# Attention, dense layer and routed experts on one core: the dense result made transposed, and routed rows kept as 16-bit planes that the DMA turns

## What is computed

```python
# attention in chunks of 64 positions: q, k, v are (4, 8, 576, 64)
scores = scale * np.matmul(q_c, k_c.transpose(0, 1, 2, 4, 3))
attn = softmax(scores)
x = np.matmul(attn, v_c)                 # as (2304, 512)
# dense layer, d_ff = 2048
h = x @ w_in
x = (h * np.clip(h + 3.0, 0.0, 6.0) / 6.0) @ w_out
# eight experts, two for each token, d_ff = 1024
noisy_logits = x @ w_gate + np.log1p(np.exp(x @ w_noise)) * noise
for e in range(8):
    for k in range(2):
        mask = top2[:, k] == e
        h = np.maximum(x[mask] @ w1[e], 0.0)
        out[mask] += top2_w[mask, k, None] * (h @ w2[e])
```

## Time and profile before

| | |
|---|---|
| median of three executions | 1008.01 us |
| the profiled execution's own time | 1007.72 us |
| its span, first to last instruction | 1005.9 us |
| TensorE clock granted, mean | 0.999 of full speed |
| TensorE busy | 978.1 us, 97% of the span |
| GpSimd busy | 481.8 us, 48% |
| VectorE busy | 466.1 us, 46% |
| ScalarE busy | 331.6 us, 33% |
| DMA | 141.31 MB, 140 GB/s mean |

### The profile page before, as it was taken

How to read it: one execution, slowest core, us unless ns; L and a number is a source line. 1 busy time by engine, 2 the same in 40 slices (tenths; PEclk the granted TensorE clock), 3 DMA queues, 4 the chain that set the end, 5 groups by cost and what they waited for, 6 DMA issues and landing times.

```text
span 1005.9 us, 18539 instructions
## 1 busy us (share of the span) xinstructions
PE 978.1 (97%) x5823; PEld 825.3 (82%) x5824; DVE 466.1 (46%) x878; ACT 331.6 (33%) x468; POOL 481.8 (48%) x743
## 2 busy tenths in 40 slices
PE   6999999999999999999999999999999999999996
PEld 6888888888988988988877878878787887888885
DVE  5554455455456456463555533433344343433344
ACT  3322333332342342332423333333333333333332
POOL 5995000100100200597562876848487584933345
PEclk9999999999999999999999999999999999999999
DMA  9352132232332322624375565656556565337629
GB/s 343 127 180 74 43 106 76 103 106 75 106 105 75 105 75 95 231 84 167 122 221 140 133 186 151 177 128 185 167 128 174 155 184 132 94 94 177 168 78 350
DMA packets 135675, 141.31 MB, mean 140 GB/s; under 512 B 96192, under 2 KB 96320, under 8 KB 135616
## 3 DMA queue, kind: packets, MB, share of 16 engines
q1 hardware_dynamic: 111376, 74.73, 25.9%
q0 software_dynamic: 12288, 44.05, 13.9%
q10 hardware_dynamic: 11952, 21.76, 7.0%
HBM read 77.07 MB, written 40.63 MB: 117 GB/s over the span
## 4 chain that ended last, share of the span: by engine, by line
PE 56%; POOL 35%; issue 4%; DMA 3%; POOLq 1%; DVE 1%; ACT 0%; SPq 0%; ACTq 0%; DVEq 0%
PE ps L1265 15%; POOL W L507 11%; PE ps L1252 11%; PE ps L1384 10%; PE ps L1279 10%; POOL W L503 8%; PE ps L1283 5%; POOL W L456 5%; POOL W L453 3%; POOL W L524 2%; POOL y_hi L544 2%; POOL W L521 1%; PE ps L1301 1%; POOL EXraw L490 1%; POOL routed_x L466 1%
## 5 line engine op out<-in xcount | busy, mean ns | idle before, releaser
L1384 PE MATMUL ps<-W,hT_part 128*128 (+1 forms) x1032 | 251.1, 398 | 2.4 <-ACT hT_part L749 1.2
L1252 PE MATMUL ps<-W,xg_part 128*128 (+1 forms) x1032 | 249.2, 396 | 4.3 <-POOLq L514 3.5
L1252 PEld LDWEIGHTS ps<-W,xg_part 128*128 128x128 f32 x1032 | 192.6, 187 | 52.9 <-issue 6.7
L1384 PEld LDWEIGHTS ps<-W,hT_part 128*128 128x128 f32 x1032 | 191.2, 189 | 45.0 <-issue 3.1
L1265 PE MATMUL ps<-x_part,W 128*128 128x384 f32 x1152 | 222.8, 342 | 3.8 <-POOL W L456 3.1
L1265 PEld LDWEIGHTS ps<-x_part,W 128*128 128x128 f32 x1152 | 200.1, 188 | 11.1 <-POOL W L456 5.4
L466 POOL DMA_INDIRECT routed_x<-x,slot_blk x36 | 36.1, 1002 | 310.8 <-DVE slot_blk L908 216.8
L507 POOL TENSOR_TENSOR W<-EXraw,W 128x256 fp32r<-128x256 f32 x224 | 164.0, 763 | 4.7
L1279 PE MATMUL ps<-W,g_part 128*128 128x512 f32 x576 | 149.9, 395 | 0.0
L503 POOL TENSOR_SCALAR W<-EXraw 128x256 fp32r<-128x256 f32 x224 | 106.5, 502 | 83.0 <-PE ps L1384 75.3
L1279 PEld LDWEIGHTS ps<-W,g_part 128*128 128x128 f32 x576 | 106.7, 188 | 17.8
(11 more groups left out here) (185 smaller groups left out, 792.3 us busy)
## 6 DMA issues: line engine op xcount, KB each, us to landing
EXraw<-in_w POOLq DMA_DIRECT2D x24, 1024.0 KB, 5.9
QKV<-qkv SPq DMA_DIRECT2D x15, 768.0 KB, 4.5
routed_y<-y_sb ACTq DMA_DIRECT2D x43, 256.0 KB, 4.7
routed_y<-zero_tile SPq DMA_DIRECT2D x14, 768.0 KB, 3.8
xg<-routed_x ACTq DMA_DIRECT2D x40, 256.0 KB, 2.9
Wraw<-w_moe SPq DMA_DIRECT2D x16, 512.0 KB, 8.2
EXraw<-in_w SPq DMA_DIRECT2D x8, 1024.0 KB, 6.3
out<-y_lo SPq DMA_DIRECT2D x18, 256.0 KB, 4.5
```

Source lines behind the costliest of these rows:

```text
L1252: last = nc.tensor.matmul(dst, a(ha), b(hb), start=(i == 0), stop=(i == n - 1))
L1384: last = nc.tensor.matmul(ps[:, 4, :], hT_part[hh][:, n, :], W[hw][:, weights(slot, W1W + n * DM, DM)], start=(n == 0 and k == 0), stop=(n ...
```

## The change

The dense layer's `down` makes x1 transposed (features x tokens): the weights become the stationary operand and g the moving one, 12 matmuls of 384 columns instead of 9 of 512, into four banks (2 to 5). Attention and gate move to banks 6 and 7. The accumulators are copied to one `x1T` (ACT two pieces of 384, DVE one of 768), and the logits read it directly; `x1_transpose` and its copies are gone. For the scatter DVE writes each tile of x1T as 16-bit planes (`halve_x1`), SP turns it by a DMA transpose (`turn_rows`), and POOL scatters the turned planes, so that `routed_x` holds planes. SP reads each expert tile from DRAM with one DMA transpose (`turn_early`, `turn_x`, two or three tiles ahead), DVE puts the planes together in `xT` (`merge_x`), and `xg_high` and `xg_low` read `xT` in SBUF; `xg_transpose`, `load_rows` and `x_residual` are gone. Tiles 0 to 2 wait for the scatters of blocks 0 to 3 alone, but the first `xg_high` waits for block 4's scatter, whose source it overwrites. g32 has one buffer. The blocks are written out in place of the loop. The gate of block 4, which runs in the last block, moves two slices forward.

```diff
-            run(0, 0, 0, 0, False, True)
-            with engine.Fori(0, (NB - 2) // 2) as w:
-                run(2 * w + 1, 1, 3 * w, 3, True, True)
-                run(2 * w + 2, 0, 3 * w, 6, True, True)
-            run(NB - 1, 1, 3 * ((NB - 2) // 2), 3, True, False)
+            for i in range(NB):
+                run(i, i % 2, 3 * ((i + 1) // 2 - 1) if i > 0 else 0, (3, 6)[i % 2 == 0] if i > 0 else 0, i > 0, i + 1 < NB)
...
+            def turn_rows(b):
+
+                src, dst = (x1T_last, x1_last) if b == NB - 1 else (x1T_halves, x1_halves)
+                if 0 < b < NB - 1:
+                    sp.wait_ge(scattered, SCATTERS * b)
+                for t in range(TB):
+                    sp.wait_ge(x1_halved, TB * b + t + 1)
+                    sp.dma_start_transpose(out=dst[t][:], in_=src[t][:].rearrange("p w n c -> p (w n c)")).then_inc(x1_turned, 16)
...
                 turn_probs(t - 1)
+                if t % TB == 1 and t > 2 * TB:
+                    turn_rows(t // TB - 2)
...
-            load_expert(0)
+            load_expert(0, range(2))
+            turn_rows(NB - 2)
+            load_expert(0, range(2, 4))
+            sp.wait_ge(scattered, SCATTERS * KNOWN)
+            sp.wait_ge(x1_turned, 16 * TB * (NB - 1))
+            turn_early(0)
             load_expert(1, range(2))
...
+            turn_early(1)
             load_expert(1, range(2, 4))
+            turn_early(2)
+            turn_rows(NB - 1)
 
             sp.wait_ge(pads_ready, 1)
             for p in range(E):
...
+            def turn_x(g):
+
+                row = sp.value_load(row_tab[0:1, bass.ds(g, 1)], min_val=0, max_val=ROWS - P)
+                sp.wait_ge(x_merged, g)
+                sp.sem_inc(wait_carrier, 1)
+                sp.dma_start_transpose(out=xT_halves[:], in_=xs[bass.ds(row, P), :]).then_inc(x_turned, 16)
...
+            sp.wait_ge(tab_ready, 1)
+            for n in range(2):
+                sp.wait_ge(scattered_late[n], SCATTERS)
+            sp.wait_ge(spare_stored, 16)
+            for g in range(EARLY, 2 * EARLY):
+                for p in range((0, 2, 3)[g - EARLY], (2, 3, E)[g - EARLY]):
+                    sp.wait_ge(padded[p], 16)
+                turn_x(g)
             for s in range(2):
                 turn_half(EARLY, s, first=True)
+            turn_x(2 * EARLY)
             with sp.Fori(EARLY + 1, GL - 1) as g:
                 for s in range(2):
                     turn_half(g, s)
+                turn_x(g + EARLY)
+            turn_x(G - 1)
...
-                            in_=x1[par][t][:, :], in_offset=None).then_inc(scattered, 16)
-                if not last:
-                    pool.wait_ge(scattered, SCATTERS * (b + 1))
-                    pool.sem_inc(x1_free, 1)
+                            in_=rows[t][:].rearrange("p n c -> p (n c)"), in_offset=None).then_inc(landed, 16)
...
-            def xg_high(g, more=True):
-                act.wait_ge(xgT_in_psum, g + 1)
-                if more:
-                    load_rows(g + 1)
-                nc.scalar.copy(xg_part[HI][:], pieces(5)).then_inc(xgh_ready, 1)
+            def xg_high(g, first=False):
+                act.wait_ge(x_merged, g + 1)
+                if first:
+                    act.wait_ge(scattered_late[0], SCATTERS)
+                else:
+                    act.wait_ge(eh_ready, g)
+                    act.wait_ge(xgl_ready, g)
+                nc.scalar.copy(xg_part[HI][:], xT[:]).then_inc(xgh_ready, 1)
...
+                nc.vector.tensor_copy(x1T[:, 2:KD, :], ps[:, ACC + 2:ACC + KD, 0:TOK]).then_inc(x1d_ready, 1)
+
+            def halve_x1(b, t):
+
+                dst = (x1T_last if b == NB - 1 else x1T_halves)[t]
+                dve.wait_ge(x1a_ready, 2 * b + 2)
+                dve.wait_ge(x1d_ready, b + 1)
+                if 0 < b < NB - 1:
+                    dve.wait_ge(x1_turned, 16 * TB * b)
+                nc.vector.tensor_copy(dst[:], x1T[:, :, t * P:(t + 1) * P].bitcast(U16).rearrange("p n (c w) -> p w n c", w=2)
+                                      ).then_inc(x1_halved, 1)
+
+            def merge_x(g):
+
+                dve.wait_ge(x_turned, 16 * (g + 1))
+                if not isinstance(g, int) or g > 0:
+                    dve.wait_ge(xgh_ready, g)
+                    dve.wait_ge(xgl_ready, g)
+                nc.vector.tensor_copy(xT[:].rearrange("p n c -> p (n c)").bitcast(U16).rearrange("p (x w) -> p w x", w=2),
+                                      xT_halves[:].rearrange("p (w n) c -> p w (n c)", w=2)).then_inc(x_merged, 1)
...
             def xg_low(g):
-                dve.wait_ge(xgT_in_psum, g + 1)
                 dve.wait_ge(xgh_ready, g + 1)
-                nc.vector.tensor_tensor(xg_part[LO][:], pieces(5), xg_part[HI][:].bitcast(F32), ALU.subtract).then_inc(xgl_ready, 1)
+                nc.vector.tensor_tensor(xg_part[LO][:], xT[:], xg_part[HI][:].bitcast(F32), ALU.subtract).then_inc(xgl_ready, 1)
...
                 halve(g, first)
                 xg_low(g + 1)
+                merge_x(g + 2)
                 merge(g)
...
-                for t in range(TB):
-                    last = nc.tensor.matmul(ps[:, 2 + t, :], g_part[LO][f % 2][:, t * P:(t + 1) * P], W[HI][:, wout],
+                for n in range(KD):
+                    last = nc.tensor.matmul(ps[:, ACC + n, 0:TOK], W[HI][:, wout + n * P:wout + (n + 1) * P], g_part[LO][f % 2][:],
                                             start=False, stop=(f == NF - 1))
...
             with pe.Fori(EARLY + 1, GL - 1) as g:
                 expert_up(g, turned=True, tell=True)
-                xg_transpose(g + 1)
                 expert_down(g - 1)
```

More of the change, by code:

```diff
@@ L244, in attention_moe_moe_program @@
         scattered = sem("scattered")
+        scattered_late = [sem(f"scattered_late{n}") for n in range(2)]
         order_step = sem("order_step")
@@ L663, in layer_block @@
                     if not attend and f == FIRST_SPLIT:
-                        xg_high(0, more=False)
+                        xg_high(0, first=True)
             act.wait_ge(zero_ready, 1)
@@ L687, in _ @@
             hidden(1)
-            xg_high(2, more=False)
+            xg_high(2)
             weight_ratio(NB - 1)
@@ L692, in _ @@
             hidden(2)
[L693 to L697 removed]
             act.wait_ge(ys_cleared, 16 * (T - TB))
[L699 removed]
             store_y(1)
[L701 to L703 removed]
+            xg_high(3)
             hidden_high(2)
@@ L730, in turned_tile @@
                 halve(g, first)
-                if first:
-                    for p in range(3, E):
-                        act.wait_ge(padded[p], 16)
                 xg_high(g + 1)
@@ L760, in _ @@
                 if g + 1 < G:
-                    xg_high(g + 1, more=g + 2 < G)
-                    xg_rest(g + 1)
+                    xg_high(g + 1)
                 if g > GL:
@@ L980, in layer_block @@
                     if gated and f == 0:
-                        take_x1(i, 1 - par)
+                        take_x1T(i)
+                    if gated and f == 1:
+                        halve_x1(i - 1, 0)
+                        halve_x1(i - 1, 1)
+                    if gated and f == 2:
+                        halve_x1(i - 1, 2)
                     if attend:
@@ L1115, in order_weights @@
                 nc.vector.tensor_tensor(wmix[:, :, 1], wmix[:, :, 1], fl[5], ALU.subtract).then_inc(wmix_ready, 1)
-            take_x1(NB, 1)
+            take_x1T(NB)
+            halve_x1(NB - 1, 0)
+            halve_x1(NB - 1, 1)
             xg_low(1)
-            gate(NB - 1, 0, 6)
+            merge_x(2)
+            gate(NB - 1, 0, ATT)
+            halve_x1(NB - 1, 2)
             hidden_low(0)
             for part in range(1, 4):
-                gate(NB - 1, part, 6)
+                gate(NB - 1, part, ATT)
             xg_low(2)
-            rows_of_block(NB - 1, 1, 6)
+            rows_of_block(NB - 1, 1, ATT)
             dve.wait_ge(slots_step, 7 * NB)
@@ L1130, in _ @@
             tile_tables()
-            gate(NB - 1, 4, 6)
+            gate(NB - 1, 4, ATT)
             result_places()
             take_y(1)
+            merge_x(3)
             xg_low(3)
             hidden_low(2)
+            merge_x(4)
             def halve(g, first=False):
@@ L1315, in ranks @@
                 last.then_inc(rank_ready, 1)
-            def xg_transpose(g):
-                pe.wait_ge(xg_loaded, 16 * (g + 1))
-                for n in range(KD):
-                    last = nc.tensor.matmul(pieces(5)[:, n, :], xg[:, n * P:(n + 1) * P], ident, is_transpose=True,
-                                            start=(n == 0), stop=(n == KD - 1), skip_group_check=True)
-                last.then_inc(xgT_in_psum, 1)
             def weights(slot, first, n):
```

228 lines of the change are left out of this document (93 added, 135 removed).

## The result

The kernel after takes 1036.03 us, median of four executions (1031.75 to 1037.52), against 1008.05 for the kernel before on the same chip: a ratio of 1.0266, 95% interval 1.0245 to 1.0288. It is slower, as forecast, but by 28 us where 12.5 was predicted, and above the range of 1000 to 1030. The profiled execution took 1037.52 us with a span of 1035.8, 29.9 us longer than the 1005.9 of before; it was the slowest of the four, 1.5 us above their median.

The account below looks back on a forecast made before the run. POOL's split was taken to set the pace in five expert periods, PE before and after. Terms -5.6 + 22.0 - 3.7 = +12.7 us on 1007.72 gave 1020.4, stated as 1020.5; range 1000 to 1030, own spread 1010 to 1030.

Parts of the forecast that it names:

- five periods: Expert-tile stretches (p = 2 to 6) paced by POOL's split, 59.04 us each before; forecast +4.4 each, +22.0 in all.
- tail: From 835.74 us, PE-bound: transposes and `x_residual` gone, -5.7; last split stretched, +2.0; net -3.7.
- Down: Dense layer's `down`: 12 matmuls of 384 columns for 9 of 512, time going by columns; difference 0.
- rival C: A fixed price per matmul makes the three more matmuls per `down` slice cost: +19, 1040 us; chance 0.02.
- x1 transposes and the end of block 5: 15 transpose groups in blocks 1 to 5 go, -6.6 us; tile 0's stall and transposes go, -2.2.
- D: Rival at the start: block 4's scatter still holds tile 0 and the gate, none of 2.2 won; a few us more.
- Tile 3: Its read queues on SP behind eight zero tiles; `expert_up(3)` at 511.4, giving back 7.5 of the 11.8 us saved.
- The splits: POOL's split per expert, 46.9 us, stretched by `xg_low`, `merge_x` and drift of gaps: +4.8, to 51.7 us.
- A: Rival: `xg_low` and `merge_x` fall in POOL's gaps or POOL goes first; -13.4, 994.6 us, faster; chance 0.20.
- Saved outside the split: 0.42 (up and down follow at 5.6 + 5.6): Per period, 0.42 us saved outside POOL's split, `expert_up` and `expert_down` taking 5.6 each; net +4.4 a period.
- the last part: Signs to look for: PE busy some 93%, waits of some 7 us for POOL's `ex_ready` five times, splits 51 to 52.
- B: Rival: SP's DMA transposes come late in the tail's 13 tiles, +15, 1036 us; chance 0.05.

Follow-up runs that it names:

- the first experiment: Kernel before plus one more DVE copy of 16-bit planes per turned tile, into scratch that nothing reads or waits for: 1021.23 us, ratio 1.0141.
- the kernel before without its lock: Kernel before, with ScalarE also writing the relu of hT to PSUM, where `turned_low` reads it instead of SBUF: 1006.24 us, ratio 0.9998.

## Why the prediction was right in sign and wrong in size

The spans differ by 29.9 us; the forecast was 12.7. By stretches, between the starts that both timelines show (us, after minus before):

| stretch | forecast | measured |
|---|---|---|
| blocks, up to tile 0 | -8.8 | -7.3 |
| tile 0 to `expert_up(1)` | -3.0 | -2.1 |
| to `expert_up(3)` | +7.5 | +8.0 |
| to the first of the five periods | -1.3 | -0.7 |
| five periods | +22.0 | +34.1 |
| tail | -3.7 | -3.6 |
| gathers, mixing, stores | 0 | +1.6 |

*Down.* Right: 0. `down` of after is 1.40 and 0.70 us, 2.10 in all. A fixed price for each matmul, rival C, would have shown here, and did not.

*x1 transposes and the end of block 5.* Right: the transposes gave 6.6 and the stall 2.2 us. Tile 0 fitted, so D is out. The 1.5 us missing from the blocks are the slow slice at 106.08.

*Tile 0 to tile 1.* Mis-sized: I counted twelve logit matmuls, but the trace has 24 records of them and they take 2.58 us, where 20 of all kinds at 0.11 were allowed. `expert_up(1)` behind them, at a lower clock (0.50 from 478.5 to 481), took 7.03 us instead of 5.7.

*Tile 3.* Right in mechanism: the eight zero tiles stood in front. `expert_up(3)` started at 514.31, against 511.4 forecast: 2.9 of the 3.4 us by which the start as a whole fell short. The landing, the merge and the high and low halves, shown below from the chain of after, cost about what the prediction gave them. SP's issue was late: the eight zero tiles took 16.01 us as before but began at 491.66, not at 488.4, and so ended at 507.67 instead of 504.4. Of these 3.3 us, 2.4 had gathered before `expert_up(1)`, and the rest came with its lower clock.

```profile
508.68 3.17 DMA xT_halves<-routed_x
511.87 0.82 DVE xT L948
512.72 0.63 ACT xg_part L656
513.37 0.70 DVE xg_part L967
...
514.31 8.05 PE ps L1306 x24
```

The tile itself took 8.05 instead of 5.86 us, after a wait of 9.9. These 2.2 us do not show in the stretch behind it (-0.7), because the stall of 1.19 went as well, which the forecast had kept, and the transposes 1.3.

*The splits.* Nearly right: +5.5 us each (46.9 to 52.4) against +4.8, so 3.5 us short over five. The price of the two instructions, 0.80 and 0.95 for the pair in the two groups shown, lies around the 0.94 taken (3.7 for the four pairs, against 3.8), and the drift of the hT merge out of POOL's gap happened as said, though in three groups where the sum took two; 0.3 more went in a longer pause ahead of one load issue (1.50 us). A, that the lock does not bite, is refuted by the trace and by the first experiment. The rule of the Trainium skill (SBUF — State Buffer, Who interferes with whom) has a copy in two-port mode hold the shared pair of ports for the whole instruction, and an instruction with two SBUF inputs contend with GpSimd's reads. It names the right instructions; 1.45 us for the pair, as if both locked for their whole length, is not what the groups show.

*The step that failed* is "Saved outside the split: 0.42 (up and down follow at 5.6 + 5.6)". The waits of some 7 us ahead of that `up` were forecast in the last part, and costed at nothing. But the first `expert_up` after such a wait runs partly at 1.2 GHz, and it is on the path, because the next split can only start once it and `expert_down` behind it are through. It took 8.12, 7.46, 8.57 and 7.76 us where 5.6 was forecast, and in the tail 7.22. Against the 5.87 of before that is +8.4 in the periods and +1.4 in the tail. PE's stall had been treated as idle time of an engine that is not the bottleneck, yet it slows PE's next work, which is on the path. The Trainium skill (TensorE: Matmul & The Clock Gate, HAM oscillation — how this bites in real kernels) describes such a loop of wait and slow start for a matmul kernel that waits for its DMA; the trace agrees, with POOL in the DMA's place (7.90 us of wait, then 7.46 for 5.59 at 669.20), and I had not drawn on it. The periods add up: 27.5 for splits, 8.4 for the clock, -1.8 for transposes outside the splits, 34.1. The forecast had saved these five times (-2.1), but between its two ends the stretch holds five splits and only four pairs of passes.

*The tail* came out right by luck: errors that cancel. The slow `expert_up(30)` cost 1.4, eleven groups of transposes and two `x_residual` went (5.3) where 5.7 was counted, one more `expert_up` took 5.85 instead of 5.60, and the stall of 2.0 forecast for the last split did not come.

*B*, late turns, did not decide: all 39.6 us that PE waits in the periods are for POOL. They showed only in the kernel before without its lock, and for the hidden tiles.

Of the 17.2 us missed, 8.4 are the clock in the periods, 3.5 the splits, 3.4 the start (with 1.5 of the clock in block 1 and 1.3 at tile 1), 1.6 the gathers, whose cause stays open, and 0.3 transposes. (The prediction's last sum adds 0.3 to 1020.4 and gives 1020.5; that slip of 0.2 changes nothing here.)

## What to carry to other kernels

An instruction that comes off the busiest engine gains only where that engine sets the pace; where it follows a slower one, ask first what the new instructions do to the slower one, down to the memory that their operands lie in. If a change leaves TensorE waiting for some microseconds, cost the matmuls behind that wait at the lower clock, above all if the next producer waits for them. And a change that loses can be one lock away from winning: beside 1006.24 for the kernel before with its own lock out, the change was worth 17 us once each subtraction of VectorE read one operand from PSUM and `merge_x` ran on ScalarE.

## What the runs showed of the hardware

- A 0.75 us VectorE copy that no engine waits for made a program of 1008 us 13 us longer: some 10 through GpSimd's split, some 3 through TensorE's clock behind its waits. One SBUF operand moved to PSUM, at the price of one more ScalarE instruction, removes the loss; with that done for both subtractions and the plane merge of x on ScalarE, GpSimd's subtracting instructions average 745 ns over the kernel, against 895 in the kernel after.
- The granted clock fell behind waits of some 8 us at every expert of the kernel after, behind waits of 3.55 to 4.14 us at all five of one kernel, and behind waits of 2.2 to 2.4 us at three of five of another, where a wait of 3.20 passed without a fall. A fall cost 1.4 to 2.7 us of one `expert_up`. With 1.13 us of dummy matmuls a tile PE had no wait for GpSimd left, and it stayed at 1.00.
- It also fell in some executions behind a burst of small matmuls in which PE is shown busy throughout (24 records in 2.58 us). After block 0, every slice whose `up` took 3 to 3.8 us in these profiles stands right behind such a burst, and most bursts have none behind them; why is open.
- A DMA transpose of one tile of 16-bit planes landed in 3.17 us from DRAM, no slower than the 3.7 us median from SBUF. From SBUF, two took 6.65 and 8.27 while GpSimd gathered.
